# Folding two weight matrices: six of eight row blocks of the first part as three products of split operands, with the opening work of all engines in another order

## What is computed

```python
for t in range(S):
    state = alpha[:, :, t, :, None] * state + np.einsum('bhd,bhe->bhde', k[:, :, t], v[:, :, t])
    y[:, :, t] = np.einsum('bhd,bhde->bhe', q[:, :, t], state)
...
h = (x @ w1) * (x @ w2) @ w3        # x 3072 x 384, w3 1024 x 1024
x = h @ w_out                       # w_out 1024 x 384
...
out += p[:, e:e + 1] * (np.maximum(x @ w1[e], 0.0) @ w2[e])
```

## Time and profile before

| What | Value |
|---|---|
| Median of 3 runs | 1222.96 us (1222.81 to 1223.23) |
| The profiled execution's own time | 1223.47 us |
| Its span, from the first to the last instruction | 1221.7 us |
| PE matmul busy | 1216.5 us (100%) |
| DVE, ACT, POOL busy | 455.4, 275.9, 169.1 us |
| First part of the fold, L1169 x80 | 28.2 us busy, mean 507 ns a row, starts 4.0 to 35.9 us |
| Second part, L1184 x48 | 16.5 us busy, mean 493 ns a row, starts 36.9 to 58.7 us |
| Mean granted TensorE clock | 1.000 |

### The profile page before, as it was taken

One profiled execution on the slowest core, in us unless ns is written; L12 is line 12 of the kernel. 1 busy time (PEld: TensorE's weight loads), 2 busy tenths in 40 slices (PEclk: granted clock), 3 DMA queues, 4 the chain that ended last, 5 costly groups with the idle time before them and its releaser, 6 DMA issues.

```text
span 1221.7 us, 18786 instructions
## 1 busy us (share of the span) xinstructions
PE 1216.5 (100%) x7710; PEld 1113.7 (91%) x7710; DVE 455.4 (37%) x874; ACT 275.9 (23%) x514; POOL 169.1 (14%) x148
## 2 busy tenths in 40 slices
PE   9999999999999999999999999999999999999999
PEld 5699999999999999999999999999999999999998
DVE  4997676676651122222222222222122222222222
ACT  1443333332333311111111111111111111111111
POOL 1032222222223530000000000000000000000000
PEclk9999999999999999999999999999999999999999
DMA  9643643643514341001141111123001111222201
GB/s 293 216 101 76 173 126 73 175 126 71 161 47 162 119 164 52 20 32 52 53 155 52 52 52 52 52 63 144 26 26 52 52 52 53 78 78 77 78 7 46
DMA packets 87542, 108.02 MB, mean 88 GB/s; under 512 B 38576, under 2 KB 57904, under 8 KB 86960
## 3 DMA queue, kind: packets, MB, share of 16 engines
q1 hardware_dynamic: 87040, 106.44, 28.1%
q10 hardware_dynamic: 432, 0.59, 0.1%
HBM read 86.29 MB, written 18.35 MB: 86 GB/s over the span
## 4 chain that ended last, share of the span: by engine, by line
PE 98%; DVE 1%; DMA 0%; issue 0%; SPq 0%; DVEq 0%; ACT 0%
PE bank L1123 32%; PE bank L1235 25%; PE bank L974 8%; PE score_banks L1235 8%; PE bank L976 8%; PE bank L975 8%; PE bank L1169 2%; PE bank L1013 2%; PE score_banks L1034 1%; PE bank L1023 1%; PE bank L1184 1%; PE score_banks L999 1%; DMA keys_t<-keys_spill 0%; PE bank L1162 0%; DMA keys_spill<-key_blocks 0%; PE score_banks L983 0%
## 5 line engine op out<-in xcount | busy, mean ns | idle before, releaser
L794 DVE SCALAR_TENSOR_TENSOR h_lo<-bank,h_hi 128x512 fp32r<-128x512 f32 x192 | 132.8, 692 | 584.4 <-ACT h_hi L586 583.6
L586 ACT ACTIVATE h_hi<-bank 128x512 fp32r<-128x512 f32 x192 | 114.7, 597 | 661.7 <-PE bank L1123 661.7
L1123 PE MATMUL bank<-x_hi,we_lo 128*128 128x512 f32 x576 | 228.7, 397 | 0.0
L1123 PE MATMUL bank<-x_hi,we_hi 128*128 128x512 f32 x576 | 224.1, 389 | 0.0
L1123 PE MATMUL bank<-x_lo,we_hi 128*128 128x512 f32 x576 | 223.5, 388 | 0.0
L1235 PE MATMUL bank<-we_hi,h_hi 128*128 128x384 f32 x576 | 194.6, 338 | 0.0
L1235 PE MATMUL bank<-we_lo,h_hi 128*128 128x384 f32 x576 | 194.5, 338 | 0.0
L1235 PE MATMUL bank<-we_hi,h_lo 128*128 128x384 f32 x576 | 193.8, 336 | 0.0
L484 POOL TENSOR_TENSOR we_lo<-we_raw,we_hi (+1 forms) x48 | 60.9, 1291 | 528.0 <-ACT we_hi L547 527.8
L1123 PEld LDWEIGHTS bank<-x_lo,we_hi 128*128 128x128 f32 x576 | 108.3, 188 | 22.7
L1123 PEld LDWEIGHTS bank<-x_hi,we_lo 128*128 128x128 f32 x576 | 108.3, 188 | 22.4
(11 more groups left out here) (89 smaller groups left out, 1442.3 us busy)
## 6 DMA issues: line engine op xcount, KB each, us to landing
x_hi<-x_hi_spill SPq DMA_DIRECT2D x24, 768.0 KB, 4.9
x_lo<-x_lo_spill SPq DMA_DIRECT2D x24, 768.0 KB, 6.3
we_raw<-wset SPq DMA_DIRECT2D x4, 3072.0 KB, 10.3
inputs<-akq SPq DMA_DIRECT2D x24, 448.0 KB, 5.1
values<-v_rows SPq DMA_DIRECT2D x24, 256.0 KB, 3.5
inputs<-akq SPq DMA_DIRECT2D x24, 224.0 KB, 3.1
x_hi_spill<-x_hi_out SPq DMA_DIRECT2D x8, 576.0 KB, 4.8
x_lo_spill<-x_lo_out SPq DMA_DIRECT2D x8, 576.0 KB, 5.6
```

What stands on the lines that cost most here:

```text
L586: act.activation(h_hi[:, s % 2, :], bank[s % 2][:, :], ACT.Relu).then_inc(h_hi_ready, 1)
L794: dve.scalar_tensor_tensor(out=h_lo[:, s % 2, :], in0=bank[s % 2][:, :], scalar=0.0, in1=h_hi[:, s % 2, :], op0=ALU.max, op1=ALU.subtract) ...
L1123: mm = pe.matmul(bank[s % 2][:, :], (we_hi if term < 2 else we_lo)[e % 2][:, cols], (x1_lo if term == 1 else x1_hi)[u][:, k, :], start=(i ...
```

## The change

Row blocks k = 2 to 7 of the fold's first part are made as split products. ACT copies each of these blocks of w_out and the first 640 columns of each of w3 to float32r (`split_high`: 384 and 640 columns), DVE subtracts the copies (`split_low`: 384 and 640 columns, the latter in place over `w3_sb`), and PE's step k waits for the two subtractions and then issues 15 matmuls in the place of five plain products. Blocks k = 0 and 1 and the whole second part stay as they are. The new tiles lie where `wb_hi` and `x0_1` come to lie later.

The rest moves work. On PE, `visit(0, 0)` goes from behind k = 6 to behind k = 7, right ahead of `turn_keys(0, 2)`, and the steps of the second part stand one or two products later. On DVE, `prepare_factors` is cut in two (keys, and queries), and the opening is written in a new order in which `split_low` stands between the attention's steps. ACT's opening and SP's order of the loads change too: the weights of blocks 3 to 7 move ahead of the queries and values, w_out's block 2 moves from ACT's queue to SP's, and SP's `turn_keys(0, 4)` moves ahead of two loads of the attention.

```diff
@@ -61,7 +61,8 @@
 PIECES = WSET // PIECE
 PARTS = 4
 FOLD_FIRST = 5
-BEGUN_BY_ACT = 3
+SPLIT_FROM = 2
+BEGUN_BY_ACT = 2
 FOLD_BANKS = [0, 1, 2, 3, 4, 0, 1, 2]
 SUM_BANKS = [5, 2, 3, 4]
 TERMS = 3
...
 
+        split = ExitStack()
+        w3_hi = sb("w3_hi", [P, FT - SPLIT_FROM, FOLD_FIRST * P], F32R, split)
+        wo_hi = sb("wo_hi", [P, FT - SPLIT_FROM, DM], F32R, split)
+        split.close()
         wb_hi = sb("wb_hi", [P, WSET], F32R, first)
...
-        x0 = [sb(f"x0_{t}", [P, CHUNKS1, KT + 1, 2, CHUNK], F32R, first) for t in range(TILES1)]
+        x0 = [sb("x0_0", [P, CHUNKS1, KT + 1, 2, CHUNK], F32R, first)]
+        split = ExitStack()
+        wo_lo = sb("wo_lo", [P, FT - SPLIT_FROM, DM], F32R, split)
+        split.close()
+        x0.append(sb("x0_1", [P, CHUNKS1, KT + 1, 2, CHUNK], F32R, first))
...
-        w3_sb = sb("w3_sb", [P, FT, FF], F32, fold)
+        raw = ExitStack()
+        w3_sb = sb("w3_sb", [P, FT, FF], F32, raw)
+        raw.close()
+        w3_lo = sb("w3_lo", [P, FT, FF], F32R, fold)
         wo_sb = sb("wo_sb", [P, FT, DM], F32, fold)
         fold.close()
...
@@ -375,13 +389,14 @@
             load_w3(2)
             sp.wait_ge(edge_set, SLOTS)
             load_keys(0, 0)
+            load_w3(3)
+            load_w3(4)
             load_queries(0, 0)
-            for k in range(3, 5):
-                load_w3(k)
+            load_w3(5)
             load_keys(0, 1)
+            load_w3(6)
+            load_w3(7)
             load_queries(0, 1)
-            for k in range(5, FT):
-                load_w3(k)
             load_keys(0, 2)
             load_queries(0, 2)
...
             move_rest(0, 2)
+            turn_keys(0, 4)
             load_queries(0, 5)
             load_keys(1, 0)
-            turn_keys(0, 4)
...
+            def split_high(k):
+                act.wait_ge(wo_loaded[k], 16)
+                act.activation(wo_hi[:, k - SPLIT_FROM, :], wo_sb[:, k, :], ACT.Copy).then_inc(split_hi, 1)
+                act.wait_ge(w3_loaded[k], 16)
+                act.activation(w3_hi[:, k - SPLIT_FROM, :], w3_sb[:, k, 0:FOLD_FIRST * P], ACT.Copy).then_inc(split_hi, 1)
...
             act.wait_ge(constants, CONSTANTS)
+            for k in range(SPLIT_FROM, 5):
+                split_high(k)
             turn_keys(0, 0)
+            split_high(5)
             check(0, 0)
+            split_high(6)
+            split_high(7)
+            turn_keys(0, 1)
             check(0, 1)
-            turn_keys(0, 1)
+            for f in range(FOLD_FIRST):
+                fold_high(f)
             x0_high(0, 0)
-            fold_high(0)
-            fold_high(1)
             turn_keys(0, 2)
-            for f in range(2, FOLD_FIRST):
-                fold_high(f)
             check(0, 2)
...
+            def prepare_key_factors(b, c):
+
...
-                dve.wait_ge(prep, base + 3)
+
+            def prepare_query_factors(b, c):
+
+                dve.wait_ge(prep, PREP_STEPS * (CHUNKS * b + c) + 3)
...
+            def split_low(k):
+                i = k - SPLIT_FROM
+                dve.wait_ge(split_hi, 2 * i + 1)
+                dve.tensor_tensor(wo_lo[:, i, :], wo_sb[:, k, :], wo_hi[:, i, :], ALU.subtract).then_inc(split_lo, 1)
+                dve.wait_ge(split_hi, 2 * i + 2)
+                at = slice(0, FOLD_FIRST * P)
+                dve.tensor_tensor(w3_lo[:, k, at], w3_sb[:, k, at], w3_hi[:, i, :], ALU.subtract).then_inc(split_lo, 1)
...
+            split_low(2)
             prepare_clamp(0, 0)
             prepare_suffixes(0, 0)
-            prepare_factors(0, 0)
+            split_low(3)
+            prepare_key_factors(0, 0)
+            split_low(4)
+            prepare_query_factors(0, 0)
+            split_low(5)
             prepare_clamp(0, 1)
             prepare_suffixes(0, 1)
+            prepare_key_factors(0, 1)
+            split_low(6)
+            split_low(7)
+            prepare_query_factors(0, 1)
             advance(0, 0)
-            prepare_factors(0, 1)
             prepare_clamp(0, 2)
             prepare_suffixes(0, 2)
-            prepare_factors(0, 2)
+            prepare_key_factors(0, 2)
+            fold_low(0)
+            prepare_query_factors(0, 2)
+            x0_low(0, 0)
             advance(0, 1)
-            fold_low(0)
-            x0_low(0, 0)
-            for f in range(1, FOLD_FIRST):
-                fold_low(f)
+            fold_low(1)
+            fold_low(2)
             prepare_clamp(0, 3)
             prepare_suffixes(0, 3)
+            prepare_key_factors(0, 3)
+            x0_low(0, 1)
             advance(0, 2)
-            prepare_factors(0, 3)
-            x0_low(0, 1)
-            fold_low(5)
+            prepare_query_factors(0, 3)
+            for f in range(3, 6):
+                fold_low(f)
             for f in range(2):
                 for i in pieces_of(f):
                     piece_low(i)
+            x0_low(0, 2)
             prepare_clamp(0, 4)
             prepare_suffixes(0, 4)
-            x0_low(0, 2)
+            prepare_key_factors(0, 4)
             fold_low(6)
             advance(0, 3)
-            prepare_factors(0, 4)
+            prepare_query_factors(0, 4)
             fold_low(7)
             g_product(0, 0)
...
-            first_beside = {3: (turn_keys, 0), 4: (first_visit, 0), 5: (turn_keys, 1), 6: (visit, 0), 7: (turn_keys, 2)}
-            second_beside = {4: (visit, 1), 10: (turn_keys, 3), 14: (visit, 2)}
+            first_beside = {3: [(turn_keys, 0)], 4: [(first_visit, 0)], 5: [(turn_keys, 1)], 7: [(visit, 0), (turn_keys, 2)]}
+            second_beside = {5: (visit, 1), 12: (turn_keys, 3), 15: (visit, 2)}
             pe.wait_ge(ones_set, 1)
             for _ in range(WARM):
                 pe.matmul(bank[7][:, 0:CHUNK], ones[:, :], ones[:, :], start=True, stop=True)
             for k in range(FT):
-                pe.wait_ge(wo_loaded[k], 16)
-                pe.wait_ge(w3_loaded[k] if k else w3_first_loaded, 16)
+                if k < SPLIT_FROM:
+                    pe.wait_ge(wo_loaded[k], 16)
+                    pe.wait_ge(w3_loaded[k] if k else w3_first_loaded, 16)
+                else:
+                    pe.wait_ge(split_lo, 2 * (k - SPLIT_FROM) + 2)
                 for f in range(FOLD_FIRST):
                     if (k, f) == (0, 1):
                         pe.wait_ge(w3_loaded[0], 16)
-                    mm = pe.matmul(bank[FOLD_BANKS[f]][:, 0:DM], w3_sb[:, k, f * P:(f + 1) * P], wo_sb[:, k, :], start=(k == 0), stop=(k == FT - 1))
+                    cols = slice(f * P, (f + 1) * P)
+                    if k < SPLIT_FROM:
+                        mm = pe.matmul(bank[FOLD_BANKS[f]][:, 0:DM], w3_sb[:, k, cols], wo_sb[:, k, :], start=(k == 0), stop=False)
+                    else:
+                        i = k - SPLIT_FROM
+                        mm = split_product(bank[FOLD_BANKS[f]][:, 0:DM], (w3_hi[:, i, cols], w3_lo[:, k, cols]),
+                                           (wo_hi[:, i, :], wo_lo[:, i, :]), False, k == FT - 1)
                     if k == FT - 1:
                         mm.then_inc(folded, 1)
                 if k == 3:
                     pe.wait_ge(constants, CONSTANTS)
-                if k in first_beside:
-                    step, c = first_beside[k]
+                for step, c in first_beside.get(k, ()):
                     step(0, c)
```

8 lines of the change are left out of this document (5 added, 3 removed).

## The result

| | before | changed |
|---|---|---|
| median | 1222.95 us (1221.95 to 1223.23, 6 runs) | 1231.46 us (1230.71 to 1232.14, 6 runs) |
| profiled execution, its span | 1223.47, 1221.7 | 1230.71, 1229.0 |
| mean granted clock of TensorE | 1.000 | 0.997 |
| PE, DVE busy | 1216.5, 455.4 us | 1214.8, 461.6 us |

The changed kernel takes 1.007 times as long (95% interval 1.0059 to 1.0081): 8.5 us slower. Forecast were 1229.3 us, from 1226.4 to 1232.2. PE is busy for only 1.7 us less, although six steps of the fold became shorter, and the span is 7.3 us longer; so PE must stand idle, and some of its work must run slower.

The account below looks back on a forecast made before the run. PE bounds the kernel (busy 1216.5 of 1221.7 us). Waits less savings gave +4.7 us, the clock +1.6: +6.3 us, 1229.8 against the profiled 1223.47, stated as 1229.3 us against the median; range 1226.4 to 1232.2.

Parts of the forecast that it names:

- first wait: Ahead of the transposes of chunk (0, 1): PE stands 5.4 us behind DVE's mask, done at 29.3 us.
- second wait: Ahead of the transposes of chunk (0, 2), right behind `visit(0, 0)`: PE idle 2.6 us for DVE's state and mask.
- third wait: Behind the first two groups of `up1`: PE idle 2.0 us for `fold_low(7)`, done at 67.7 us.
- clock: PE's clock falls in the wait ahead of the second transposes and returns during steps 6 and 7: 1.6 us.
- wait for `keys_t`: At the visit at 65.33 us, PE's wait for keys read back by DMA goes away: -0.8 us.
- PE's work: Six fold steps of 15 split matmuls in place of five plain products save 4.1 us.
- likeliest case: Slower by waits of PE for DVE and one fall of the clock: 1229.3 us, chance 0.43.
- a second time: Rival: clock falls longer or again, or DVE's new operations cost more: +8 to +9 us, 1231.5, chance 0.20.
- PE's price for a split product: In the fold's split steps: 0.176 us a matmul, so 15 cost 2.64 us against 3.33 for five plain products.
- DVE's price: A pair of subtractions for one row block costs DVE 1.34 us, six pairs 8.0.
- DVE's order ahead of the first mask: First transposes at 17.2 us, `split_low(5)` done at 19.9, then DVE's queue up to the mask at 29.3.
- The port: DVE operations with two SBUF inputs exclude POOL's: a clash could add up to 1 us; counted at nothing.

Follow-up runs that it names:

- third_wait_back: The changed kernel with DVE's clamp and suffixes of (0, 4) ahead of `x0_low(0, 2)`, and `fold_low(7)` ahead of the scans of (0, 4): 1229.51 us.
- visit_back: The changed kernel with `visit(0, 0)` put back on PE behind step 6 of the fold: 1236.0 us.
- fill_first_wait: The changed kernel with 19 useless 128x128 products on PE during the wait ahead of the second transposes: 1231.37 us.
- mask_before_splits: The changed kernel with DVE's `advance(0, 0)` put ahead of the subtractions of blocks 6 and 7 and the scans for chunk 1: 1229.94 us.
- order_alone: The changed kernel's order without splits: all eight row blocks by plain products, no copies or subtractions for them: 1229.47 us.
- visit_and_mask_back: The changed kernel with `visit(0, 0)` back behind step 6 and DVE's `advance(0, 1)` ahead of `fold_low(0)`: 1229.34 us.
- second_back_first_filled: visit_and_mask_back with 19 useless 128x128 products added on PE in the wait ahead of the second transposes: 1227.2 us.

## Why the prediction was right, and where it was off

The sum, as the prediction made it (+6.3 us against the profiled execution), beside what the change's trace shows (+7.3):

| step | forecast | trace |
|---|---|---|
| first wait | 5.4 | 4.70 |
| second wait | 2.6 | 3.17 |
| third wait | 2.0 | 1.89 |
| clock | 1.6 | 1.56 + 1.51 = 3.1 |
| wait for `keys_t` | -0.8 | -0.82 |
| PE's work | -4.1 | -4.7 (what remains) |

The forecast's own sum by starts was 0.4 lower than its terms added up, as it said. The last row is not measured: it is what is left of the 7.3.

- **Direction and mechanism** came out: PE, on which everything hangs, saved its four microseconds and stood behind DVE for ten (4.70 + 3.17 + 1.89 = 9.8). The likeliest case was right in kind; by its clock the result is the rival's in which it falls "a second time" (1231.5).
- **The mis-sized term is the clock.** The prediction took one fall behind the first wait, 1.6 us. That one cost 1.56, and this closeness is luck: 1.6 was picked between 0 and 5.3, and in third_wait_back and visit_back the same fall costs 2.0 and 2.1. But the second wait brought another, 1.51, which was left to a rival because at 2.6 us it seemed short of the 3.0 of the earlier trace rows; at 3.17 it was not. The granted clock of 42 to 46 us, 0.57, is the row. The Trainium skill ("TensorE: Matmul & The Clock Gate", HAM oscillation) says that idle gaps of PE drop the clock and each return is paid for anew, and the trace agrees, twice (0.60 and 0.57).
- **PE's price for a split product** was right: steps 6 and 7 at full clock with the transposes take 5.74 us in fill_first_wait, 2.69 a step with 0.36 for the transposes (forecast 2.64). The 0.6 us that remain beyond 4.1 are most likely no gain of the change: in its profiled execution the first 20 records of the fold took 7.09 us, in those of the other kernels with splits 7.07 to 8.32 for the same instructions. That execution was also the fastest of the six.
- **DVE's price** was a little high (1.34 a pair, 1.26 measured). **DVE's order ahead of the first mask** was right but for the start. The first transposes came at 16.09, not 17.2; ACT copies block 5 right behind them, and DVE, which had waited 1.26 us for that copy, was done with the block at 19.1, not 19.9. The rest of the way took some 0.5 us less than counted, so the mask was done at 28.06, not 29.3.
- **The second wait had half of its reason, and a term too small.** The prediction let DVE start its state and mask when the visit was over, and they did start then (37.89 against 37.88). But DVE's queue had the fold's first result, the scans and `x0_low(0, 0)` in front, and `x0_low(0, 0)`, which needs the output of that same visit, ends with it in this order. So two reasons meet, and visit_back, which takes away the visit alone, made things worse. The prediction did not ask here what it asked of the third wait: what is queued on DVE in front of the operation waited for. The size was 0.6 short because it took `advance(0, 0)`'s 2.55 us: from the second chunk on the state is also decayed (L799 and L792 above, 0.48 from start to start), and `advance(0, 1)` took 3.0, as the earlier trace rows show for `advance(0, 3)`. With those 3.04 us (55.02 to 58.06) the wait would have come out at the 3.0 of the earlier trace rows and not short of it, and there would have been no reason to leave the second fall out of the sum.
- **The third wait and `keys_t`** were right to a tenth, and third_wait_back gives back just what the wait takes.
- **The port** stood at nothing, and in the change's trace it is nothing: none of DVE's scans and subtractions beside the fold is longer there than its like. Elsewhere it was up to the 1 us that the prediction named. In visit_back and four other kernels a subtraction starts some 0.35 us before POOL's first turn ends and takes 0.77 us instead of 0.56, 0.21 more. In mask_before_splits the two operations shown above start 1.11 and 0.84 us before POOL's turn ends and take 0.97 and 0.71 more. In all three DVE loses what was left of POOL's operation less some 0.14 us, so it seems to stand still until POOL is nearly done. In the change POOL's first turn (16.48 to 17.77) ends 0.11 us after the subtraction of block 5 has started, and that takes its usual 0.56.

## What to carry to other kernels

When an edit makes the bottleneck engine's work shorter and another's longer, write out the other's queue up to each thing that the first one waits for: here 4.1 us were saved on PE, and an order that kept what PE waits for behind work which nobody needed yet cost 9.8, and 3.1 more by the clock. Move first what somebody waits for, at every such place, since one wait mended alone gave most of its time to the next; and split only as much as the helping engine has free time for: four blocks gained where six gave it all back. And count an idle gap of three microseconds on PE at more than its length, since the clock fell behind each such gap here, and once behind one of 1.9 us, and cost 1.2 to 2.8 us more; useless products in the gap kept the clock up in both kernels that had them, which was worth 2.1 us at the median in one and nothing in the other, where a second gap was left open.

## What was unexpected of the hardware

- The clock fell behind every wait of 3.16 us or more in the profiled executions (ten waits in seven kernels, the change among them); behind the third wait, 1.9 us, it fell in one of seven, visit_back, and behind none that was shorter. What a fall costs varies for the same code: from the transposes behind the second wait to the next visit 4.57 us at the full clock, and 5.78, 6.08, 6.08, 6.09, 7.08 and 7.36 in visit_back, the change, order_alone, third_wait_back, mask_before_splits and fill_first_wait. How long the clock stayed low explains most of it. In stretches of 0.25 us it is low for about 3.5 us in the first four kernels of this list (in the change from 42.25 to 46.0; in visit_back from 44.5, before the wait was over) and for about 7 us in mask_before_splits and fill_first_wait (39.5 to 46.5). Behind the first wait it is the same: short in the change and visit_and_mask_back (1.56 and 1.43 us lost), long in third_wait_back and visit_back (1.98 and 2.10). What makes a low stretch short or long was not found.
- A late start is passed on to PE over two other engines. Before the mask that the second transposes wait for, DVE works off its row from block 5 on; ACT's copy of block 5 stands behind the first transposes; and these stand behind the fold's first four steps, which wait for weights to land. In the change, visit_and_mask_back, third_wait_back, fill_first_wait, visit_back and second_back_first_filled the first transposes start at 16.09, 16.36, 16.37, 16.94, 17.34 and 17.45 us, for the same instructions up to there, and the second ones at 28.21, 28.53, 28.50, 29.11, 29.94 and 30.13, each 12.1 to 12.7 us later. DVE's first subtraction, which waits for w_out's block 2, starts between 8.42 and 10.12 us in these traces. The kernel before has waits for the weights too and none for a subtraction; its runs spread by 0.7 to 3.5 us, by comparison (those two left out). That the landing and the clock together make the spread is argued, not shown.
